# Sums read back behind the loads, inverted a step earlier, and maxima, DMA issues and scores reordered in a bucketed-attention kernel

## The reference

```python
q_bits = (np.einsum('bhsd,dk->bhsk', q, proj) > 0)
k_bits = (np.einsum('bhsd,dk->bhsk', k, proj) > 0)
q_bucket = np.sum(q_bits * powers, axis=-1)        # the same for k
mask = q_bucket[:, :, :, None] == k_bucket[:, :, None, :]
scores = np.where(mask, scale * q @ k.T, -1e9)
scores = scores - np.max(scores, axis=-1, keepdims=True)
attn = np.exp(scores)
attn = attn / (np.sum(attn, axis=-1, keepdims=True) + 1e-09)
out = attn @ v                                     # then x: (1536, 512)
x = prelu(x @ w_in1) @ w_out1                      # 512 -> 2048 -> 512
x = (P(h) / (Q(h) + 1e-6)) @ w_out2, h = x @ w_in2 # rational activation
```

## Time and profile before

| | |
|---|---|
| median of 3 runs | 804.44 us (803.89 to 805.59) |
| the profiled execution | 804.27 us, span of its instructions 802.2 us |
| granted TensorE clock, mean | 0.998 of 2.4 GHz |
| busy: PE, DVE, ACT, POOL | 97%, 66%, 45%, 35% of the span |
| attention stage | 0 to about 271 us |
| the two layers | about 271 us to the end, PE busy 527.1 of 531.2 us |

### The profile page before, as it was taken

One profiled execution on the slowest core, in us unless ns is written; L12 is line 12 of the kernel. 1 busy time (PEld: TensorE's weight loads), 2 busy tenths in 40 slices (PEclk: granted clock), 3 DMA queues, 4 the chain that ended last, 5 costly groups with the idle time before them and its releaser, 6 DMA issues.

```text
span 802.2 us, 11727 instructions
## 1 busy us (share of the span) xinstructions
PE 780.0 (97%) x3820; PEld 583.7 (73%) x3820; DVE 530.7 (66%) x822; ACT 357.7 (45%) x588; POOL 281.4 (35%) x341
## 2 busy tenths in 40 slices
PE   8899999999998999999999999999999999999998
PEld 5456556565565678888888888887888888888886
DVE  6877667676772654345333533379888988888886
ACT  7344554554454310112111201157667666676673
POOL 7565664664864579400000077781000000000000
PEclk9999999999999999999999999999999999999999
DMA  4676675675582144100000033330000100000001
GB/s 126 166 185 162 159 186 138 156 195 130 149 206 47 54 150 119 41 1 0 1 1 14 0 92 92 100 94 3 1 1 1 53 1 1 1 18 35 1 1 52
DMA packets 34206, 58.85 MB, mean 73 GB/s; under 512 B 9900, under 2 KB 13780, under 8 KB 34164
## 3 DMA queue, kind: packets, MB, share of 16 engines
q1 hardware_dynamic: 31796, 53.15, 24.6%
q10 hardware_dynamic: 2368, 5.15, 2.6%
HBM read 29.59 MB, written 3.24 MB: 41 GB/s over the span
## 4 chain that ended last, share of the span: by engine, by line
PE 76%; DVE 6%; POOL 5%; issue 5%; DMA 4%; SPq 3%; ACT 1%; POOLq 0%; DVEq 0%; ACTq 0%
PE ps_h L1316 32%; PE acc L1348 32%; DMA work<-rden_scratch 3%; PE ps_o L584 3%; PE ps_a L499 2%; PE ps_s L554 2%; PE ps_s L559 2%; DVE row_max L1015 1%; DVE p_sum L1048 1%; PE ps_o L605 1%; POOL v_three L932 1%; POOL x_lo L946 1%; POOL lo L855 1%; PE ps_a L495 1%; DMA den<-den_scratch 1%
## 5 line engine op out<-in xcount | busy, mean ns | idle before, releaser
L1381 ACT ACTIVATE g_hi<-num 128x512 fp32r<-128x512 f32 x96 | 60.0, 625 | 207.6 <-PE acc L1348 203.3
L1451 DVE TENSOR_TENSOR g_lo<-num,g_hi 128x512 fp32r<-128x512 f32 x96 | 72.3, 753 | 78.7 <-ACT g_hi L1381 78.1
L726 ACT ACTIVATE p<-ps_s 128x768 f32<-128x768 f32 x96 | 77.6, 811 | 83.9 <-PE ps_s L559 61.4
L1015 DVE TENSOR_REDUCE row_max<-ps_a 128x1 f32<-128x384 f32 x180 | 92.0, 553 | 31.6 <-PE ps_a L499 29.0
L1316 PE MATMUL ps_h<-x_hi,w_late_in_hi 128*128 128x512 f32 x288 | 78.9, 394 | 0.0
L1316 PE MATMUL ps_h<-x_hi,w_late_in_lo 128*128 128x512 f32 x288 | 78.8, 394 | 0.0
L1316 PE MATMUL ps_h<-x_lo,w_late_in_hi 128*128 128x512 f32 x288 | 78.8, 394 | 0.0
L584 PE MATMUL ps_o<-p,v_use 128*64 128x384 f32 x384 | 74.5, 507 | 0.0
L1459 DVE TENSOR_SCALAR num<-ps_h,alpha_sb 128x512 f32<-128x512 f32 x48 | 36.0, 750 | 54.4 <-PE ps_h L1316 52.6
L1389 ACT ACTIVATE den_q<-ps_h,abs_b 128x512 f32<-128x512 f32 x48 | 33.0, 688 | 83.7 <-PE ps_h L1316 77.5
L1048 DVE TENSOR_TENSOR p_sum<-p 128x768 f32<-128x768 f32 x48 | 54.2, 1133 | 14.8 <-PE ps_o L605 9.9
(11 more groups left out here) (166 smaller groups left out, 1557.6 us busy)
## 6 DMA issues: line engine op xcount, KB each, us to landing
stage<-in_w_in SPq DMA_DIRECT2D x26, 256.0 KB, 2.7
stage<-in_w_out SPq DMA_DIRECT2D x26, 256.0 KB, 2.8
raw<-in_qk SPq DMA_DIRECT2D x15, 384.0 KB, 3.9
q<-hi SPq DMA_DIRECT2D x30, 192.0 KB
k<-hi SPq DMA_DIRECT2D x30, 192.0 KB
v_raw<-in_v SPq DMA_DIRECT2D x16, 192.0 KB, 3.8
work<-rden_scratch SPq DMA_DIRECT2D x16, 192.0 KB, 3.5
out<-y SPq DMA_DIRECT2D x12, 256.0 KB, 2.5
```

What stands on the lines that cost most here:

```text
L726: nc.scalar.activation(halves(p[c][:]), ps_s[c % 2][:, :, 0:HALF], ACT.Exp, scale=float(D) ** -0.5).then_inc(s_exp, 1)
L1015: dve.tensor_reduce(row_max[slot][:, i, c:c + 1], ps_a[:, i, 0:HALF], AX.X, ALU.max).then_inc(s_a_free, 1)
L1381: nc.scalar.activation(g_hi[f % 2][:], num[f % 4][:], ACT.Copy).then_inc(s_ghi, 1)
L1451: dve.tensor_tensor(g_lo[f % 2][:], num[f % 4][:], g_hi[f % 2][:], ALU.subtract).then_inc(s_glo, 1)
```

## The change

It reorders instructions, and computes the same.

- In `uses_of` (TensorE and VectorE), chunk 2 of the maxima goes from between the scores of steps 2 and 3 to behind both; chunk 3 stays behind the values.
- SyncE, all heads but the first: `fill_stats` and `store_sums` come ahead of `load_raw` and `load_v`, and `turn_sums` ahead of `fill_a_pen` and `stage_early`.
- TensorE, head 0 only: the second head's first two score chunks go behind the values of steps 4 and 5.
- ScalarE: `fill_a_hi`'s two DMA issues go behind the exponential of the next step (but not in head 0), `x_high` from the start of step 4 to the end of step 3.
- VectorE: `reciprocals` goes from behind the last group of the first head to behind the middle one.

```diff
--- before.py
+++ after.py
@@ -290,8 +290,8 @@
                 more, bits = left > 0, left > 1 or (left == 1 and u == 0)
                 return [([("a", 2, 0)] if more else [], [("a", 2, 1)] if more else []),
                         ([("m", 1, 0)] + ([("bits", 3, 0)] if bits else []), []),
-                        ([("a", 2, 2)] if more else [], [("a", 2, 3)] if more else []),
-                        ([], []),
+                        ([], [("a", 2, 3)] if more else []),
+                        ([("a", 2, 2)] if more else [], []),
                         ([("a", 2, 4)] if more else [], []),
                         ([("a", 2, 5)] if more else [], [])]
 
@@ -452,20 +452,23 @@
                     for u in range(2):
                         h = 2 * j + u
                         first = isinstance(j, int) and j == 0
-                        if left > 1:
+                        if first and u == 0:
                             load_raw(u, j + 2)
-                        if left:
                             load_v(u, j + 1)
+                        if left or u == 0:
+                            fill_stats(1 - u, j + u)
                         if not (first and u == 0):
                             store_sums(sp, 1 - u, j - 1 + u, h - 1, den_row[1 - u][:])
-                        if left or u == 0:
-                            fill_stats(1 - u, j + u)
+                        if left > 1 and not (first and u == 0):
+                            load_raw(u, j + 2)
+                        if left and not (first and u == 0):
+                            load_v(u, j + 1)
+                        if u == 0 and not first:
+                            turn_sums(sp, j - 1)
                         if left > 1 or (left == 1 and u == 0):
                             fill_a_pen(1 - u, h + 3)
                         if left == 1:
                             stage_early(2 + u)
-                        if u == 0 and not first:
-                            turn_sums(sp, j - 1)
                         if left:
                             fill_b_hi(u, j + 1)
                         if u == 0 and not first:
@@ -658,7 +661,7 @@
                                 t = KC * h + c
                                 if c + 2 < KC:
                                     scores(u, j, c + 2, t + 2)
-                                elif not (final and u == 1):
+                                elif not (first or (final and u == 1)):
                                     scores(1 - u, j + u, c + 2 - KC, t + 2)
                                 for kind, g, cc in steps[c][0]:
                                     at = (u + g) % 2, j + (u + g) // 2
@@ -680,6 +683,9 @@
                                 values(u, h, c, KC * h + c)
                                 if c == 3:
                                     empty_rows(u, h)
+                                if first and c + 2 >= KC:
+
+                                    scores(1, 0, c + 2 - KC, c + 2)
                             for c in range(begin, begin + group):
                                 for kind, g, cc in steps[c][1]:
                                     at = (u + g) % 2, j + (u + g) // 2
@@ -817,8 +823,6 @@
                             t = KC * h + c
                             if c == (3 if first and u == 0 else 1) and not (last or (first and u == 1)):
                                 stat_rows(1 - u, j + u)
-                            if c == 4 and u == 1 and not first:
-                                x_high(act, j - 1)
                             if c + 2 < KC:
                                 exponential(c + 2, h, t + 2)
                             elif not last:
@@ -829,9 +833,12 @@
                                 stat_rows(0, 1)
                             if c == (4 if first and u == 0 else 2) and (left > 1 or (left == 1 and u == 0)):
                                 split_qk(1 - u, j + 1 + u)
+                            if c == (4 if first and u == 0 else 3) and (left > 1 or (left == 1 and u == 0)):
                                 fill_a_hi(1 - u, h + 3)
                             if c == 3 and not last:
                                 copy_v(1 - u, j + u)
+                            if c == 3 and u == 1 and not first:
+                                x_high(act, j - 1)
                         if last:
 
                             act.wait_ge(s_xlo, PAIRS - 1)
@@ -1122,7 +1129,7 @@
                                             maxima(*at, n)
                                 if side == 0 and (begin + group) % 2 == 0:
                                     add((begin + group) // 2 - 1, h)
-                            if begin == 4 and u == 0 and not first:
+                            if begin == 2 and u == 0 and not first:
                                 reciprocals(dve, j - 1)
 
                 over_pairs(dve, pair)
```

## The result

| | before | after |
|---|---|---|
| median | 804.16 us (802.52 to 805.59, 4 runs) | 816.64 us (811.40 to 819.82, 4 runs) |
| profiled execution | 804.27 us, span 802.2 | 819.82 us, span 817.7 |
| granted TensorE clock, mean | 0.998 | 0.974 |

The changed kernel takes 1.0149 times as long, 95% interval 1.0092 to 1.0207. Its four runs differ with the clock: 811.4 us at a mean of 0.987, 819.8 at 0.974.

The account below looks back on a forecast made before the run. TensorE was taken to bound the kernel, its second-head turns waiting for GpSimd's late `mcols`. -3.6 + 2.2 - 0.3 - 2.0 - 1.6 + 0.2 = -5.1 us gave 799.3 us, range 792.5 to 803.5.

Parts of the forecast that it names:

- Second heads: Loop's second heads: `normalise` starts 0.9 us earlier, the addition holds GpSimd 0.8, turn at T+15.5; five heads -3.6 us.
- What happens when both run is in pair 6: Precedent for second heads: at 219.55 VectorE's addition took 2.53 us instead of 0.96, ending 0.8 behind the split's end.
- (b): Rival, loop heads: additions are passed over between back-to-back GpSimd operations, as at 49.34; 805.8 us, chance 0.08.
- the 1.4 us stands of the loop: TensorE's waits at second heads' turns: the run's mean clock left no room for a second large clock fall behind them.
- First heads: Loop's first heads: addition 1 asked for 0.13 us behind GpSimd's split, head 0.45 us longer; five times, +2.2 us.
- (a): Rival, loop's first heads: VectorE's addition gets in ahead of GpSimd's split; 794.1 us, chance 0.25.
- (c): Rival: the readback lands late and VectorE stands between chunks 3 and 4, 0.6 us in six heads; 802.9 us, chance 0.07.
- (d): Rival: the broadcast did not hold GpSimd, `normalise` stays, only pair 6 gains and first heads lose; 802.9 us, chance 0.05.
- -0.3: Pair 6, first head, outside the loop: the readback goes ahead of two weight loads that delayed the inversion; -0.3 us.
- -2.0: Pair 6, second head: the broadcast comes 3 us earlier, so the head takes 13.6 us instead of 15.66; -2.0 us.
- -1.6: Behind pair 6's last turn: without the 2.18 us stand the clock stays up; 1.7 us, counted as -1.6.
- First pair: Second head's first scores moved behind the values: bounds -1.1 and +0.9 us, taken as +0.2.

Follow-up runs that it names:

- e12: The changed kernel with a GpSimd wait for `pen` complete ahead of `normalise` (first four loop pairs), none behind it: 802.98 us, 1.0002.
- e1: The changed kernel with GpSimd waiting in second heads for its own `normalise` to complete before the split: 802.00 us, 0.9972.
- e2: The changed kernel with eight zero matmuls where TensorE stands for VectorE in second heads: 804.07 us, 1.0011.
- e3: The kernel before with only the order of the maxima changed: 807.54 us, 1.0049.
- e4: The kernel before with only SyncE's order and the earlier inversion changed: 799.77 us, 0.9947.
- e7: The changed kernel with head 0's order as before: 814.49 us, 1.0116.
- e10: The changed kernel with five tiny GpSimd additions ahead of `normalise`, so that it begins later: 828.07 us, 1.0303.
- e13: The changed kernel with ScalarE's copy of `hi` in second heads ahead of the exponential: 822.44 us, 1.0242.
- e5: e4 with ScalarE's moved DMA issues and a GpSimd wait for its own `normalise` ahead of the split: 799.45 us, 0.9941.
- e6: The kernel before with only head 0's order changed: 805.09 us, 1.0015.
- e9: e3 with four tiny VectorE reductions ahead of the second head's first addition, so that it is asked for later: 808.95 us, 1.0061.
- e11: e5 with eight zero matmuls ahead of the last turn: 799.12 us, 0.9938.
- e8: The changed kernel with a useless 128x6 GpSimd addition between `normalise` and split, no wait added: 809.38 us, 1.0078.

## Why the prediction was wrong

**The step that failed** is in *Second heads*: "What happens when both run is in pair 6", with which the addition was to get in between `normalise` and the split, held 0.8 us. It was held 2.3 us, for the whole of the split (3.29 us less its own 0.96). The row it rests on is right, but its split had itself begun behind a stand, `[0.66 <-ACT hi L704]` at 219.55. In the loop `normalise` had one too, 0.97 us for the broadcast, and that stand is what the change removes. The row that spoke for (b), 49.34, had no stand ahead: `pen` began there straight behind the split of a weight.

```profile
46.84 1.28 POOL L922 TENSOR_TENSOR w_early_out_lo<-stage,w_early_out_hi 128x512 fp32r<-128x512 f32 x1
48.08 1.46 POOL L864 TENSOR_TENSOR pen<-bit,cst 24x768 fp32r<-24x768 f32 x1
```

Once GpSimd ran `pen`, `normalise` and split back to back, VectorE was not let in between. e12 shows it from the other side: given a stand of 0.31 us, second heads are 15.5. That this is the forecast's number is partly luck, since `normalise` begins at T+5.96 there and not at T+5.75; in e1, where it begins at T+5.62 and the addition is let in, they are 15.2.

**Rival (b)** had this mechanism and "a gain of 0 for 3.6". It had a chance of 0.08, and two things were off. In first heads it didn't hold: their split stands 1.07 us for ScalarE, and the addition beside it was 2.60 us, let in at the first boundary as forecast. And it priced a second head at 16.2; with the clock up that is 16.0 (e2). The remaining 12.6 us of these five heads are TensorE's clock. The text took the 1.4 us stands of the loop as a sign that such a stand costs no clock, and one of those was even longer:

```profile
151.17 0.32 PE L510 MATMUL ps_a<-ident,mcols 128*120 128x128 f32 x1 [1.58 <-POOL mcols L913]
```

No fall follows it. The new stand of 1.56 us, in another place of the head, did cost clock. No rival carried a second price of that kind, and so the range ended at 803.5.

**Both edits were needed** (e3, e4, e7): the readback makes GpSimd run back to back, which holds the addition; the order of the maxima has TensorE arrive earlier at the half that it then waits for. It is let go at T+10.59 in both kernels, and comes at T+9.03 after and at T+9.63 in e4, hence 1.56 us instead of 0.96. That these two edits are enough without ScalarE's two moves isn't shown: every kernel with a fall in each second head (after, e7, e10, e13) has those moves too.

**First heads**, +2.2 forecast, +2.1 measured, by the steps given: addition asked behind the split (by 0.05 us, forecast 0.13), heads of 15.22. In e4 and e5, without the edit, they are 14.80: in first heads it only cost. Rivals (a) and (c) didn't come: VectorE was second, and no inversion waited, the readback landing in 2.2 us in the median and 2.8 at most, where (c) took 5.4. Nor (d).

**Pair 6.** -0.3 became -0.39. The -2.0 became -0.7, since the broadcast was still late there: `normalise` began 0.9 us earlier in the head (T+6.62, before T+7.55) where the text had the broadcast 3 us earlier. GpSimd stood 2.19 us for it, not 3.53, and the turn 1.88, not 2.18.

```profile
250.00 2.10 POOL L948 TENSOR_TENSOR work<-o_sb,work 128x768 f32<-128x768 f32 x1 [2.19 <-DMA work<-rden_scratch]
```

So the fall of the clock stayed (259.8, 3.4 us), and the -1.6 with it; behind it a stand of 1.2 us of TensorE for GpSimd's `w_late_in_lo` (line 1287) was new, about as much as the +1.15 of the last part. The profiled executions of before and e4 don't have it, and its cause stays open. e4's turn came at 14.95 too.

**First pair.** +0.2 became +1.84, outside the bounds of the text. The other kernels' first pairs tell two causes apart. Without the head 0 edit and without a fall of the clock the pair ends at 57.75 to 57.97 (before, e4, e5, e7), with the edit and no fall at 58.38 to 58.83 (e2, e6, e12): the edit costs 0.4 to 1.1 us. With a fall near 34 us it ends at 59.02 to 59.93 without the edit (e3, e9, e11) and at 59.32 to 60.10 with it (after, e1, e8, e10, e13). So the fall, 6.8 us long in after, isn't the edit's, and with the edit a pair with a fall that long is 1 us or more longer than one without. With e6's 0.5 for the edit that is the larger part of the miss; the sum had no term for it.

The Trainium skill, "SBUF — State Buffer" (Who interferes with whom), says that issue order decides which of VectorE and GpSimd waits, and that the later one is blocked while the other's instruction runs. The length of each hold agrees: in all that are shown here the addition began to run, 0.96 us before its end, within 0.2 us of the end of a GpSimd instruction. But an addition asked for 0.64 us before the split began (115.77, 116.41) ran behind it, so by order of begin alone it would have gone first.

## What to carry to other kernels

When an edit takes away an engine's wait, ask what that wait let happen: here a stand of 1 us on GpSimd was where VectorE got its turn, and a cheap completion wait put back at either boundary (e1, e12) won back 12 to 14 us by the ratios, though only to the kernel before (0.9972 and 1.0002). Take a row as precedent only with the bracket behind it, since what released the instruction may be what made the case. And price a new stand of TensorE twice, once as itself and once at half the clock behind it.

## What the runs showed of the hardware

- **GpSimd run back to back keeps VectorE out over several operations.** Two-input additions of VectorE (128x768, 0.96 us alone), asked for during `normalise`:

| kernel | `normalise` stood | asked after its start | addition | let in |
|---|---|---|---|---|
| after | no | 1.16 | 3.29 | behind the split |
| e4, last four | no | 0.77 | 3.67 | behind the split |
| e4, first | 0.42 | 0.31 | 2.36 | behind `normalise` |
| e8 | no | 1.15 | 3.44 | behind the split, two boundaries missed |
| e10 | no | 0.40 | 5.82 | behind `x_lo` (in the first one even later) |
| e13 | no | 1.15 | 5.04 | behind `x_lo` |
| e3 | 1.00 | 0.12 | 2.55 | behind `normalise` |
| e12 | 0.31 | 0.81 | 1.85 | behind `normalise` |
| e9, four of five | 0.74 to 0.92 | 0.48 to 0.66 | 2.0 to 2.2 | behind `normalise` |
| e1 | no, but the split stood 0.22 | 1.14 | 1.51 | behind `normalise` |

  In after and e4 `x_lo` had to wait (0.20 and 0.98 us) and the addition came in there, as it did in e8, where 0.07 us lie between the split's end and `x_lo`; in e10 and e13 it hadn't and was passed ahead too. At the boundary to the value sums (`v_three`, 128x192) the addition was mostly let in, behind a back-to-back operation too (123.43 in e10), but not always: in e10's first second head it was passed ahead there as well.

```profile
81.39 6.33 DVE L1058 TENSOR_TENSOR p_sum<-p 128x768 f32<-128x768 f32 x1
...
86.33 0.58 POOL L940 TENSOR_TENSOR v_three<-v_raw 128x192 f32<-128x192 f32 x1
86.98 0.92 POOL L942 TENSOR_TENSOR v_part<-v_three 128x64 f32<-128x64 f32 x1
```

  What the arbitration looks at stays open. A stand ahead of the running operation, or at its end, decides at the boundary from `normalise` to the split; how it does so, no run shows.
- **TensorE's clock behind short stands.** A stand of 1.56 us was followed by 6.8 us at 1.2 GHz in four second heads and by 3.4 us in the fifth; eight matmuls of 320 columns (1.34 us) ahead of it, which left 0.42 us, prevented all five. Stands of 1.71 us in e8's second heads were followed by one fall in five, those of 3.3 us in e13's by one of 6.8 us and four of 3.4, those of 0.96 us in e4's by none.
